# Transposes one step later, later ranking stages, an earlier x split, and cluster rows moved and partly made on ScalarE, in a fused attention and two-MLP kernel

## The chip, the cores and the metric

The kernel runs on one core of one Trainium2 chip. The metric is the device time of one execution in microseconds; three runs of the kernel before gave 794.3, 794.31 and 795.95. TensorE is called PE in the profile, VectorE DVE, ScalarE ACT, GpSimd POOL and SyncE SP.

## The reference, cut to what matters

Attention runs on 2 batches of 8 heads with 768 tokens and head size 64. Each query and key is given to the cluster (of 16) whose normalised centroid it is nearest to; a query sees only keys of its own cluster. The 1536 tokens then pass two MLPs in fp32.

```python
q_assign = argmax(q_n @ c_n)          # k_assign likewise, per head
scores = where(q_assign == k_assign, scale * q @ k.T, -1e9)
attn = softmax(scores) @ v
h = x @ w_in                          # x: attention output, 1536 x 512; w_in 512 x 2048
g = P(h) / Q(h)                       # P cubic, Q = 1 + |b0||h| + |b1|h^2
x2 = g @ w_out                        # 2048 x 512
out = (silu(x2 @ w_gate) * (x2 @ w_val)) @ w_out2
```

## The kernel before, in words

Every fp32 operand is split into a high part that the matmul takes exactly and a low part (the rest), and products are summed from two or three matmuls.

**Steps.** The attention phase is one loop over steps, from -18 to 107, written out on all five engines. Step i makes the scores of tile i: head i // 6, 128 queries by 768 keys (96 tiles in all). The other stages of a tile follow some steps later. Within one step TensorE goes through: scores of tile i (L1226, L1229), the six transposes of tile i - LAG (L1239), the PV matmuls of a group (L1254, L1256), the transposes of is_top (L1278), the rank matmul (L1292), one half of a head's centroid logits (L1313), and from step 96 to 103 half a unit of the first MLP's hidden product (L1109 to L1111, asked for by TAIL_CHUNKS). A group is three tiles; its PV runs in three steps, beginning at PV_LAG = LAG + 3 behind its first tile.

**VectorE in a step:** at some steps the cluster rows (L1024, L1026), the row maximum neg_max (L1035), every third step the sums row_den and reciprocals row_inv of three tiles (L1046, L1049), the low parts probT_lo of the transposed tile (L1057, two halves), at the end of a group x_raw (L1066), and the stages of the next head: logit sum and top (L1072, L1074), is_top (L1080). **ScalarE in a step:** exp of tile i - 1 (L811), the copy topT (L819), the high parts probT_hi (L829, two halves), x_part at the end of a group (L839), logit_lo (L861). **POOL:** normalisation of three tiles (L589), the splits of q and k (L597 to L606), of v (L614, L617), of MLP weights (L624, L626), and of a finished pair of heads x (L636, L638).

**What ties them.** The transposes of a tile write the two PT banks of PSUM, so they wait until probT_lo of the tile before has read each half (s_pT_lo), and for the normalisation (s_norm). The first PV matmul of a group waits for the low parts of its last tile and for x_raw of the group before (s_xsum). The maximum waits for the scores, exp for the maximum, and the scores of tile i for exp of tile i - 2.

**Head stages.** `head_at(step, stage)` says which head is in a stage: step = 6 h - 18 + stage + late. Stages are the split (0), logits (6 and 7), their sum (8), is_top (9), its transpose (10), the rank matmul (11) and the cluster rows (12). The rank matmul gives, for each query and key, -0.5 in the row of its first best centroid and 0 or more elsewhere. The cluster rows are made of it: 1 or 0 for q, -2^96 or 0 for k. SP sends them in six transfers per head to qk_low (L390), where they are part of the score matmul's operands. The logits and the rank product lie in one PSUM bank, so the logits of the next head wait for the cluster rows (s_cluster).

**The end of attention.** TAIL puts the activation of hidden units 0 and 1 into steps 98 and 100, on ScalarE (hidden_read, L685 to L693), VectorE (mlps, L925 to L953) and POOL (mlp1, L516); TAIL_LOG puts their logarithm and the high part g_hi (hidden_finish, L711 to L726) into steps 99 and 101. The first result matmul, first_result(0), follows the loop and waits for the last x_raw, since its results take the attention's PSUM banks. In a step, each engine does the attention's work ahead of this.

Of the kernel before, what the change touches and what calls it, by code (L numbers as in the profile page):

```python
# [21 lines left out]
def build_program(nc, q, k, v, centroids, w_in, w_out1, a, b, w_gate, w_val, w_out2, out):  # L22
    P = 128
# [5 lines left out]
    T = S // P  # L29
# [185 lines left out]
    def sem(name):  # L215
        return nc.alloc_semaphore(name)
# [22 lines left out]
        "s_pT", "s_pT_hi", "s_pT_lo", "s_pv", "s_xhi", "s_xlo"))  # L239
    s_w1p_hi, s_w1p, s_w1hi, s_w1lo = (sem(x) for x in ("s_w1p_hi", "s_w1p", "s_w1hi", "s_w1lo"))  # L240
# [16 lines left out]
    LAG = 5  # L257
    PV_LAG = LAG + HALF
    V_STEP = 3
    X_STEP, LAST_X_STEP = 5, 2  # L260
# [7 lines left out]
    def head_at(step, stage):  # L268


        for h in range(NH):
            late = -4 * (h == 1) + (h == 2 and stage <= S_SUM)
            if T * h + late == step + PREP_LEAD - stage:
                return h
        return None

    def tile_at(step):
        return step if 0 <= step < NT else None
# [85 lines left out]
    with block:  # L364

        @block.sync
        def _(sp):
# [19 lines left out]
            def send_cluster(h):  # L387
                sp.wait_ge(s_cluster, 2 * h)
                for t in range(T):
                    sp.dma_start(*cluster_rows(h, t)).then_inc(s_clrows[h % 3], 16)  # L390
# [88 lines left out]
        def _(pool):  # L479
# [103 lines left out]
            for step in STEPS:  # L583
# [45 lines left out]
                if pv_at(step - LAST_X_STEP) == (NG - 1, HALF - 1):  # L629
                    g1, third = NG - 1, HALF - 1  # L630
# [27 lines left out]
        def _(sc):  # L658
# [144 lines left out]
            for step in STEPS:  # L803

                i = tile_at(step - 1)
# [68 lines left out]
        def _(ve):  # L874
# [136 lines left out]
            for step in STEPS:  # L1011
# [8 lines left out]
                elif h is not None:  # L1020
                    ve.wait_ge(s_rank, h + 1)
                    if h > 1:
                        ve.wait_ge(*clustered(h - 1))
                    v_.tensor_scalar(clusterT[0:T * C, 0, :], rank_out[0:T * C, 0:P], 0.0, 1.0,  # L1024
                                     ALU.is_lt, ALU.mult).then_inc(s_cluster, 1)
                    v_.tensor_scalar(clusterT[0:T * C, 1, :], rank_out[0:T * C, P:2 * P], 0.0, -BIG,  # L1026
                                     ALU.is_ge, ALU.mult).then_inc(s_cluster, 1)
                i = tile_at(step)
                if i is not None:

                    ve.wait_ge(s_score, i + 1)
                    if i >= T:
# [3 lines left out]
                                     ALU.max, negate=True).then_inc(s_max, 1)  # L1036
                if (step - HALF) % HALF == 0 and 0 <= (step - HALF) // HALF < NG:
# [61 lines left out]
        def _(pe):  # L1099
# [110 lines left out]
            for step in STEPS:  # L1210
# [85 lines left out]
                for n in range(2):  # L1296
# [9 lines left out]
                    if h == 0:  # L1306
                        pe.wait_ge(s_cen, 1)
                    elif h > 1:
                        pe.wait_ge(s_cluster, 2 * (h - 1))
# [67 lines left out]
```

## Time and profile before

| | |
|---|---|
| median of three runs | 794.31 us |
| the profiled execution | 794.28 us |
| its span, first to last instruction | 792.5 us |
| TensorE busy | 781.2 us (99%) |
| VectorE busy | 571.9 us (72%) |
| ScalarE busy | 517.3 us (65%) |
| POOL busy | 522.7 us (66%) |
| granted TensorE clock, mean | 0.996 of full |

A row of a timeline gives the start in us from the span's start, the duration, the engine, the line, the operation, and the tile written and those read with their shapes; x6 means six instructions merged into one row. In brackets stands the idle time of the engine before the row and what ended it. Matmuls overlap in the pipeline and their ends are modelled, so their start times are what can be trusted. PEld is the load of weights, SPq the time in which SP issues a transfer.

### The profile page before, as it was taken

The numbers are of one execution on the slowest core, as the hardware profiler recorded it, in microseconds if no ns is written. First come the engines' busy times: TensorE is split into PE (matmuls) and PEld (weight loads), VectorE is DVE, ScalarE is ACT, GpSimd is POOL, SyncE is SP. The second block draws the span as 40 slices with busy tenths as digits, with TensorE's granted clock in tenths as the row PEclk, the third lists the DMA queues.
The fourth block names the chain that finished last, engine by engine and source line by source line (L and its number), as shares of the span: only waits on it lengthen the run. The fifth ranks groups of instructions, "written<-read, shape, count | busy, mean of one in ns | idle before, by whom it ended". The sixth has DMA issues, their size and how long they took to land.

```text
span 792.5 us, 12617 instructions
## 1 busy us (share of the span) xinstructions
PE 781.2 (99%) x4204; PEld 697.7 (88%) x4204; DVE 571.9 (72%) x1043; ACT 517.3 (65%) x957; POOL 522.7 (66%) x457
## 2 busy tenths in 40 slices
PE   8999999999999999999999999999999999999998
PEld 7799999999998888888888888899999999999997
DVE  5899999999997888778777777745445545554453
ACT  4888888888887787777767889744444444333322
POOL 4767988998575799322222288888889876655620
PEclk8999999999999999999999999999999999999999
DMA  8776555454310700000000011241111114111102
GB/s 206 180 199 162 143 140 125 116 145 121 85 60 19 221 28 0 1 1 1 1 1 0 1 55 54 66 147 50 32 54 53 37 45 134 54 28 53 28 1 80
DMA packets 57681, 57.92 MB, mean 73 GB/s; under 512 B 6608, under 2 KB 44304, under 8 KB 57616
## 3 DMA queue, kind: packets, MB, share of 16 engines
q1 hardware_dynamic: 57376, 56.52, 26.6%
q8 instruction: 34, 0.56, 0.3%
q10 hardware_dynamic: 240, 0.59, 0.3%
q14 instruction: 31, 0.25, 0.1%
HBM read 33.59 MB, written 3.15 MB: 46 GB/s over the span
## 4 chain that ended last, share of the span: by engine, by line
PE 87%; DVE 8%; issue 2%; ACT 2%; DMA 0%; DVEq 0%; ACTq 0%
PE ps L1111 18%; PE ps L1109 18%; PE ps L1110 18%; PE ps L1239 6%; PE ps L1204 4%; PE ps L1205 4%; PE ps L1203 4%; DVE neg_max L1035 3%; DVE probT_lo L1057 3%; PE ps L1254 3%; PE ps L1226 3%; PE ps L1256 3%; PE ps L1313 2%; PE ps L1229 2%; ACT prob L811 1%
## 5 line engine op out<-in xcount | busy, mean ns | idle before, releaser
L516 POOL TENSOR_TENSOR den<-den,mag 128x512 f32<-128x512 f32 x48 | 62.3, 1298 | 121.8 <-ACT den L689 121.6
L1111 PE MATMUL ps<-x_hi,w_lo 128*128 128x512 f32 (+1 forms) x384 | 139.5, 363 | 0.0
L1109 PE MATMUL ps<-x_hi,w_hi 128*128 128x512 f32 (+1 forms) x384 | 139.4, 363 | 0.0
L1110 PE MATMUL ps<-x_lo,w_hi 128*128 128x512 f32 (+1 forms) x384 | 139.3, 363 | 0.0
L575 POOL TENSOR_TENSOR w_lo<-w_raw,w_hi 128x768 fp32r<-128x768 f32 (+1 forms) x48 | 101.6, 2125 | 56.4 <-ACT w_hi L742 56.4
L589 POOL TENSOR_SCALAR prob<-prob,row_inv 128x768 f32<-128x768 f32 x96 | 85.6, 907 | 39.2 <-DVE row_inv L1049 38.7
L829 ACT ACTIVATE probT_hi<-ps 128x384 fp32r<-128x384 f32 x192 | 84.2, 489 | 25.9 <-PE ps L1239 24.2
L1057 DVE TENSOR_TENSOR probT_lo<-ps,probT_hi 128x384 fp32r<-128x384 f32 x192 | 96.8, 545 | 5.3 <-ACT probT_hi L829 4.0
L1035 DVE TENSOR_REDUCE neg_max<-ps 128x1 f32<-128x768 f32 x96 | 91.1, 950 | 8.8 <-PE ps L1229 8.5
L811 ACT ACTIVATE prob<-ps,neg_max 128x768 f32<-128x768 f32 x96 | 86.8, 905 | 10.8 <-DVE neg_max L1035 10.1
L1239 PE MATMUL ps<-ident,prob 128*128 128x128 f32 x576 | 81.7, 277 | 4.4 <-DVE probT_lo L1057 4.1
L1239 PEld LDWEIGHTS ps<-ident,prob 128*128 128x128 f32 x576 | 65.6, 140 | 17.0 <-issue 9.9
L1109 PEld LDWEIGHTS ps<-x_hi,w_hi 128*128 128x128 f32 x384 | 72.1, 188 | 8.2
L1110 PEld LDWEIGHTS ps<-x_lo,w_hi 128*128 128x128 f32 x384 | 72.1, 188 | 8.2
L1111 PEld LDWEIGHTS ps<-x_hi,w_lo 128*128 128x128 f32 x384 | 72.1, 188 | 7.5
L1111 PE MATMUL ps<-g_hi,w_lo 128*128 128x512 f32 x192 | 74.8, 390 | 0.0
L1110 PE MATMUL ps<-g_lo,w_hi 128*128 128x512 f32 x192 | 74.8, 390 | 0.0
L1109 PE MATMUL ps<-g_hi,w_hi 128*128 128x512 f32 x192 | 74.8, 390 | 0.0
L1254 PE MATMUL ps<-probT_hi,v_split 128*128 128x384 f32 x192 | 72.5, 378 | 0.0
L763 ACT ACTIVATE act_hi<-ps 128x384 fp32r<-128x384 f32 x48 | 23.6, 492 | 64.6 <-DVE ps L992 43.7
L1256 PE MATMUL ps<-probT_lo,v_split 128*128 128x384 f32 x192 | 64.6, 337 | 0.0
L959 DVE TENSOR_TENSOR sum<-ps,gate 128x384 f32<-128x384 f32 x24 | 13.4, 557 | 68.9 <-PE ps L1111 68.9
(145 smaller groups left out, 1987.5 us busy)
## 6 DMA issues: line engine op xcount, KB each, us to landing
k_hihi<-qk_hi SPq DMA_DIRECT2D x32, 192.0 KB, 4.0
w_raw<-in_moe_w_gate SPq DMA_DIRECT2D x48, 128.0 KB, 2.3
w_raw<-in_moe_w_val SPq DMA_DIRECT2D x48, 128.0 KB, 2.5
w_raw<-in_moe_w_in SPq DMA_DIRECT2D x16, 256.0 KB, 3.7
w_raw<-in_moe_w_out SPq DMA_DIRECT2D x16, 256.0 KB, 5.0
qk_raw<-in_q SPq DMA_DIRECT2D x16, 192.0 KB, 3.4
q_hilo<-qk_hi SPq DMA_DIRECT2D x16, 192.0 KB, 3.4
qk_low<-qk_hi SPq DMA_DIRECT2D x16, 192.0 KB, 4.5
```

The source lines that it names most:

```text
L575: did(g.tensor_tensor(lo[:, wave, :], raw[:, wave, :], hi[:, wave, :].bitcast(F32), ALU.subtract), s_w2lo)
L589: did(g.tensor_scalar(prob[i][:, :], prob[i][:, :], row_inv[:, i:i + 1], 1.0, ALU.mult, ALU.mult), s_norm)
L811: s.activation(prob[i % T][:, :].rearrange("p (c n) -> p c n", c=2), ps[:, bank:bank + 2, 0:HC], ACT.Exp, bias=neg_max[:, i % T:i % T + 1] ...
L829: s.activation(probT_hi[g % 2][:, n * HALF:(n + 1) * HALF, c:c + P], ps[:, PT_BANK + n, 0:HC].rearrange("p (k n) -> p k n", k=HALF), ACT.C ...
L1035: v_.tensor_reduce(neg_max[:, i % T:i % T + 1], ps[:, bank:bank + 2, 0:HC], AX.XY, ALU.max, negate=True).then_inc(s_max, 1)
L1057: v_.tensor_tensor(probT_lo[g % 2][:, keys, c:c + P], ps[:, PT_BANK + n, 0:HC].rearrange("p (k n) -> p k n", k=HALF), probT_hi[g % 2][:, k ...
L1109: mm(dst, hi, m_hi, start=start, stop=False)
L1110: mm(dst, hi, m_lo, start=False, stop=False)
L1111: return mm(dst, lo, m_hi, start=False, stop=stop)
L1239: last = transpose(ps[:, PT_BANK + n, kt % HALF * P:(kt % HALF + 1) * P], prob[i % T][:, kt * P:(kt + 1) * P], ident[:, :])
L1254: mm(ps[:, O_BANK, 0:HC], vv, probT_hi[g % 2][:, kt, :], start=(kt == 0), stop=False)
L1256: last = mm(ps[:, O_BANK, 0:HC], vv, probT_lo[g % 2][:, kt, :], start=False, stop=(kt == T - 1))
```

## The change

LAG goes from 5 to 6: the transposes, the high and low parts and PV of each tile come one step later, and the loop has one step more. For heads 2 and later, the stages from the logits on come one step later than 6 h - 18 + stage (for head 2 that was so up to the logit sum), and the split keeps its step. The x pairs are split one step after their last PV, where it was five (two for the last pair). The q cluster rows are made by ScalarE as Relu(-2 x), ahead of exp, with a new semaphore s_qrow; the k rows stay on VectorE, but behind the maximum of the step, and wait for s_qrow. s_cluster now counts one per head. Nothing else in the loop is changed; TAIL, TAIL_LOG and TAIL_CHUNKS keep their steps.

```diff
--- before.py
+++ after.py
@@ -237,6 +237,7 @@
         "s_score", "s_max", "s_exp", "s_den", "s_inv", "s_norm"))
     s_pT, s_pT_hi, s_pT_lo, s_pv, s_xhi, s_xlo = (sem(x) for x in (
         "s_pT", "s_pT_hi", "s_pT_lo", "s_pv", "s_xhi", "s_xlo"))
+    s_qrow = sem("s_qrow")
     s_w1p_hi, s_w1p, s_w1hi, s_w1lo = (sem(x) for x in ("s_w1p_hi", "s_w1p", "s_w1hi", "s_w1lo"))
     s_w2sum, s_w2hi, s_w2lo, s_wohi, s_wolo = (sem(x) for x in (
         "s_w2sum", "s_w2hi", "s_w2lo", "s_wohi", "s_wolo"))
@@ -254,10 +255,10 @@
 
     R_LAG = 3
     COPIES, CLROWS = 16 * 6, 16 * T
-    LAG = 5
+    LAG = 6
     PV_LAG = LAG + HALF
     V_STEP = 3
-    X_STEP, LAST_X_STEP = 5, 2
+    X_STEP = 1
     PREP_LEAD = 18
     FIRST_STEP = -PREP_LEAD
     S_SPLIT, S_CEN, S_LOGIT, S_SUM, S_TOP, S_TOPT, S_RANK, S_CLUSTER = 0, 2, 6, 8, 9, 10, 11, 12
@@ -269,7 +270,9 @@
 
 
         for h in range(NH):
-            late = -4 * (h == 1) + (h == 2 and stage <= S_SUM)
+            late = -4 * (h == 1)
+            if h >= 2:
+                late = 1 if stage >= S_LOGIT else int(h == 2)
             if T * h + late == step + PREP_LEAD - stage:
                 return h
         return None
@@ -385,7 +388,7 @@
                     sp.dma_start(dst, src).then_inc(s_copy[h % 3], 16)
 
             def send_cluster(h):
-                sp.wait_ge(s_cluster, 2 * h)
+                sp.wait_ge(s_cluster, h)
                 for t in range(T):
                     sp.dma_start(*cluster_rows(h, t)).then_inc(s_clrows[h % 3], 16)
 
@@ -626,8 +629,6 @@
                     did(g.tensor_tensor(w1_lo[u][:, :], w1_raw[u][:, :], w1_hi[u][:, :].bitcast(F32),
                                     ALU.subtract), s_w1p)
                 g1, third = pv_at(step - X_STEP)
-                if pv_at(step - LAST_X_STEP) == (NG - 1, HALF - 1):
-                    g1, third = NG - 1, HALF - 1
                 if third == HALF - 1 and g1 % 4 == 3:
                     pool.wait_ge(s_xsum, g1 + 1)
                     finish_last()
@@ -802,6 +803,13 @@
 
             for step in STEPS:
 
+                h = head_at(step, S_CLUSTER)
+                if h:
+                    sc.wait_ge(s_rank, h + 1)
+                    if h > 1:
+                        sc.wait_ge(*clustered(h - 1))
+                    s.activation(clusterT[0:T * C, 0, :], rank_out[0:T * C, 0:P], ACT.Relu, scale=-2.0
+                                 ).then_inc(s_qrow, 1)
                 i = tile_at(step - 1)
                 if i is not None:
                     sc.wait_ge(s_max, i + 1)
@@ -1017,14 +1025,6 @@
                         v_.tensor_scalar(qk_low[0][0:C, g, :].rearrange("c (t n) -> c t n", t=T)[:, cols, :],
                                          rank_rows[:, cols, g, :], 0.0, worth, op, ALU.mult
                                          ).then_inc(s_row0, 1)
-                elif h is not None:
-                    ve.wait_ge(s_rank, h + 1)
-                    if h > 1:
-                        ve.wait_ge(*clustered(h - 1))
-                    v_.tensor_scalar(clusterT[0:T * C, 0, :], rank_out[0:T * C, 0:P], 0.0, 1.0,
-                                     ALU.is_lt, ALU.mult).then_inc(s_cluster, 1)
-                    v_.tensor_scalar(clusterT[0:T * C, 1, :], rank_out[0:T * C, P:2 * P], 0.0, -BIG,
-                                     ALU.is_ge, ALU.mult).then_inc(s_cluster, 1)
                 i = tile_at(step)
                 if i is not None:
 
@@ -1034,6 +1034,11 @@
                     bank = score_bank(i)
                     v_.tensor_reduce(neg_max[:, i % T:i % T + 1], ps[:, bank:bank + 2, 0:HC], AX.XY,
                                      ALU.max, negate=True).then_inc(s_max, 1)
+                h = head_at(step, S_CLUSTER)
+                if h:
+                    ve.wait_ge(s_qrow, h)
+                    v_.tensor_scalar(clusterT[0:T * C, 1, :], rank_out[0:T * C, P:2 * P], 0.0, -BIG,
+                                     ALU.is_ge, ALU.mult).then_inc(s_cluster, 1)
                 if (step - HALF) % HALF == 0 and 0 <= (step - HALF) // HALF < NG:
 
                     half = (step - HALF) // HALF
@@ -1306,7 +1311,7 @@
                     if h == 0:
                         pe.wait_ge(s_cen, 1)
                     elif h > 1:
-                        pe.wait_ge(s_cluster, 2 * (h - 1))
+                        pe.wait_ge(s_cluster, h - 1)
                     centers = cenT[:, h % H, :, :].rearrange("p n c -> p (n c)")
                     for t in range(n * HALF, (n + 1) * HALF):
                         for x in (qk_hi, qk_lo):
```

## Rows read from the trace of the kernel before

**Rows 1.** TensorE's timeline over a head in mid-attention: start us, us, engine line op out<-in

```profile
101.83 0.82 PE L1239 MATMUL ps<-ident,prob 128*128 128x128 f32 x6
...
104.57 0.82 PE L1239 MATMUL ps<-ident,prob 128*128 128x128 f32 x6
...
106.63 0.82 PE L1239 MATMUL ps<-ident,prob 128*128 128x128 f32 x6
...
109.05 0.92 PE L1239 MATMUL ps<-ident,prob 128*128 128x128 f32 x6 [0.21 <-DVE probT_lo L1057]
...
113.75 0.91 PE L1239 MATMUL ps<-ident,prob 128*128 128x128 f32 x6
...
115.03 0.19 PEld L1313 LDWEIGHTS ps<-cenT,qk_hi 128*128 128x128 f32 x1
```

**Rows 2.** VectorE's timeline, of a head before and of the same head

```profile
97.20 0.94 DVE L1035 TENSOR_REDUCE neg_max<-ps 128x1 f32<-128x768 f32 x1
98.29 1.02 DVE L1057 TENSOR_TENSOR probT_lo<-ps,probT_hi 128x384 fp32r<-128x384 f32 x2
...
112.05 0.96 DVE L1035 TENSOR_REDUCE neg_max<-ps 128x1 f32<-128x768 f32 x1
113.04 1.02 DVE L1057 TENSOR_TENSOR probT_lo<-ps,probT_hi 128x384 fp32r<-128x384 f32 x2
113.98 0.28 DVE L1024 TENSOR_SCALAR clusterT<-ps 96x128 fp32r<-96x128 f32 x1
...
114.37 0.94 DVE L1035 TENSOR_REDUCE neg_max<-ps 128x1 f32<-128x768 f32 x1
115.24 0.15 DVE L1046 TENSOR_REDUCE row_den<-row_sum 128x3 f32<-128x6 f32 x1
...
115.51 0.99 DVE L1057 TENSOR_TENSOR probT_lo<-ps,probT_hi 128x384 fp32r<-128x384 f32 x2
```

**Rows 3.** ScalarE's timeline in the same head

```profile
112.10 0.37 ACT L819 ACTIVATE topT<-ps 96x256 fp32r<-96x256 f32 x1
112.37 0.86 ACT L829 ACTIVATE probT_hi<-ps 128x384 fp32r<-128x384 f32 x2
```

**Rows 4.** SyncE's queue in the same head: one issue line for six transfers

```profile
103.27 3.88 SPq L390 DMA_DIRECT2D qk_low<-clusterT  x6
```

**Rows 5.** VectorE's and TensorE's timelines at the start of attention

```profile
22.70 0.94 DVE L1035 TENSOR_REDUCE neg_max<-ps 128x1 f32<-128x768 f32 x1
...
28.71 0.92 PE L1239 MATMUL ps<-ident,prob 128*128 128x128 f32 x6
```

**Rows 6.** timelines of TensorE, ScalarE and VectorE at the end of attention, steps 95 to 99

```profile
240.92 0.82 PE L1239 MATMUL ps<-ident,prob 128*128 128x128 f32 x6
...
243.05 0.92 PE L1239 MATMUL ps<-ident,prob 128*128 128x128 f32 x6 [0.47 <-DVE probT_lo L1057]
...
248.64 0.82 PE L1239 MATMUL ps<-ident,prob 128*128 128x128 f32 x6
...
249.92 0.61 ACT L685 ACTIVATE mag<-ps 128x512 f32<-128x512 f32 x1
...
253.46 1.01 DVE L1057 TENSOR_TENSOR probT_lo<-ps,probT_hi 128x384 fp32r<-128x384 f32 x2
```

**Rows 7.** timelines of VectorE and TensorE from step 100 to the first result

```profile
256.92 0.69 DVE L925 SCALAR_TENSOR_TENSOR den<-den,ps 128x512 f32<-128x512 f32 x1
...
260.42 0.68 DVE L953 TENSOR_TENSOR g_lo<-ps,g_hi 128x512 fp32r<-128x512 f32 x1
...
261.29 0.33 PE L1254 MATMUL ps<-probT_hi,v_split 128*128 128x384 f32 x1
...
262.70 0.56 DVE L1066 TENSOR_TENSOR x_raw<-ps,x_part 64x384 f32<-64x384 f32 x1 [1.59 <-ACT x_part L839]
...
263.41 0.47 PE L1109 MATMUL ps<-g_hi,w_hi 128*128 128x512 f32 x1
```

**Rows 8.** groups of instructions by line, ScalarE: count, busy us, mean ns, idle before

```profile
L663 ACT ACT_TABLE_LOAD x1 | 1.3, 1283 | 1.4 <-PEq L1358 1.4
```

## The prediction

> **What bounds the kernel now.** I read the page first. It shows TensorE busy nearly all the time, but matmul ends are modelled, so that number hides waits of some tenths of a us; only start times show them. So I took the timelines of TensorE, VectorE and ScalarE over one head of attention, then the start and the end of attention. From the first result matmuls of the hidden layer on, nothing is touched by the change, and those 529 us stay.
>
> In attention each step starts its six transposes at a time that I call T. A plain step costs TensorE 2.06 us (104.57 to 106.63), one with half of a head's logits 2.74 (101.83 to 104.57) [rows 1]. The two steps from 104.57 to 109.05 take 4.48 where TensorE has 4.12 of work: the row at 109.05 says that the transposes wait for VectorE, whose low halves (probT_lo) free their PSUM bank. A head takes 14.7 us, of which I count 14.0 as TensorE's work (six plain steps 12.4, logits 1.4, an estimated 0.3 for the transposes and the product of the ranking). So 0.7 per head, at most 9 us in 13 regular heads, could be won. VectorE sets the time in the four steps with the logit sum, is_top and both x_raw; TensorE sets it in the two with the logits (T = 113.75 and the next). A saving helps only in the first kind, a late signal hurts in both.
>
> **The change, as places.** LAG 6 and the later head stages both shift by one step, so transposes, PV, logits, top and rank keep their order against one another: a step of after looks like the step before it in the old kernel. What moves against this pattern is the scores and maxima (one tile ahead), the row sums with their reciprocals, and the cluster rows. I number the places by the old step modulo 6: T = 113.75 is place 0, T = 109.05 place 4.
>
> **Row sums** (two small VectorE instructions, 0.27 us, 115.24 to 115.51 [rows 2]) leave places 0 and 3 for 5 and 2. From 3 to 2 they stay on the same VectorE stretch, the 4.48: nothing. From 0, where TensorE sets the time, to 5, where VectorE does: a cost. At place 5 the low half starts 0.99 behind the maximum (112.05 to 113.04) in one parity of heads and 1.09 (97.20 to 98.29) in the other; maximum and row sums together take 0.87 (114.37 to 115.24) and 0.27, that is 1.14 [rows 2]. So 0.15 and 0.05, mean 0.10. In 13 heads 1.3 us. In the last two heads, where VectorE sets every step, the sums use up small waits for ScalarE: I estimate -0.3.
>
> **Cluster rows.** Both leave VectorE's place 0 (0.39, 113.98 to 114.37 [rows 2]). They are covered there by the logits, so taking them away gives nothing. ScalarE's Relu reads 96x128. No row shows it; nearest is ScalarE's 96x256 copy, which holds the engine 0.27 (112.10 to 112.37 [rows 3]). I take 0.27, ends 0.2 (VectorE's price) and 0.45. It stands behind the rank matmul and ahead of an exponential, which comes up to 0.4 later; the scores that need it come 2 us behind it: nothing on the path. If that cover is gone, 0.4 per head.
> The k rows now come behind the maximum, and the next head's logits wait for them (s_cluster). With the low half started at 113.04, VectorE is free at 113.98, has the maximum at 114.85, the k rows (0.28) at 115.13 and the signal at about 115.23 [rows 2]. TensorE loads the first logit weights at 115.03 [rows 1], 0.20 too early. Part of that is hidden, since weights are loaded ahead of the matmul that uses them, while the last PV matmul still runs: I take 0.13 per head, ends 0 and 0.3. In 13 heads: 1.7 us.
>
> The Trainium skill, "ScalarE: Activation LUTs", section "Rules for kernel authors", says to do relu on VectorE and not on ScalarE. By that rule the q rows would be dearer after the change, as the rows put it too (0.27 against 0.2); the sum is the same by either, since neither price lies on the path.
>
> **x pairs.** POOL makes them three steps earlier, off the step in which they delay the next normalisation, and the transposes come one step later behind that. POOL isn't what TensorE waits for now, so nothing won; nothing lost either, since each group of three steps on POOL becomes shorter or stays. If they still delayed a normalisation, it has a step of 2.3 more.
> **SP.** The six cluster transfers go out from 103.27 on, 3.9 us, although their rows were ready near 99.7: copies are ahead of them [rows 4]. The scores that read them come near 113, 5.9 later than the last issue; the change takes one step of 2.3 of that. Nothing; if the rest is used up by landing, up to 1 us per head.
>
> **Start.** Step 3 loses is_top to step 4, so maximum 4 starts at 22.30 and not at 22.70 [rows 5]. Then by the prices above: maximum 0.95, exponential 1.02, signal 0.08, scores 0.90: maximum 6 at 25.25; with row sums (1.14) to 26.39; low half 0.94 to 27.33; maximum 0.87, k rows 0.28, signal 0.12: logits at 28.60; logits and scores 1.37: T of tile 2 at 29.97. Before: 28.71 [rows 5]. Cost 1.3, bounds 0 and 2.
>
> **End,** the largest term. The diff leaves TAIL, TAIL_LOG and TAIL_CHUNKS where they are, while transposes and PV end one step later.
> (1) T of step 96 in after has place 95 of before, 240.92. From step 96 to 98: 5.59 as before (243.05 to 248.64) [rows 6].
> (2) In step 98 ScalarE now has x_part ahead of the first hidden read. x_raw, behind x_part, starts 1.41 after its PV group (261.29 to 262.70 [rows 7]), PV 0.57 to 0.65 after T. So the read starts at T+2.06, where it was T+1.28 (248.64 to 249.92). From the read to the low half of the step after 3.54 (249.92 to 253.46) [rows 6], 0.54 for its first part, 0.13 signal: T of step 100 comes 6.27 behind that of step 98, 0.75 more than TensorE needs.
> (3) In step 100 VectorE does the activation of n=1, 4.2 us (256.92 to 260.42 plus 0.68) [rows 7]. Before, no low half was left behind it. Now tile 95's is, and then x_raw, and the last group's first PV waits for both: low half of tile 94 done at T+2.07, activation to 6.27, low half 1.0, x_raw 0.56, signal 0.15: T+7.98. TensorE is there at T+5.53: a wait of 2.45.
> (4) Two PV groups with their hidden chunks, 2.1 each, then the last PV group, behind which no chunk is left. Before, a chunk covered the way x_part, x_raw, first result (261.29 to 263.41, 2.12) [rows 7]; now 1.43 of that is open.
> Sum: 5.59 + 6.27 + 7.98 + 2.1 + 2.1 + 2.12 = 26.15; before 263.41 - 240.92 = 22.49. The open waits are 4.6, and 1.0 goes that before had around step 96 (the row at 243.05 shows 0.47 of it [rows 6]). Cost 3.7; bounds 1.4 (only (4)) and 5.
>
> **Sum:** 1.3 + 1.3 - 0.3 + 1.7 + 3.7 = 7.7 us. The profiled execution took 794.28 (span 792.5 and 1.8 around it), the median of the runs is 794.31, so no correction. Forecast 802.0.
>
> **Rivals.**
> A. The steps of attention come out even: late k rows and row sums fall into slack that I misread by 0.2 us. Start and (4) alone give 794.3 + 1.3 + 1.4 = 797.0, with the whole end 799.3. For it: both costs are near the length of a signal. Chance 0.20.
> B. Faster. The wait at 109.05 is not for the low halves but for POOL's normalisation, or VectorE's full queue as a whole, and the extra step with 0.2 us less VectorE per head dissolves it: 0.37 x 14 = 5.2 won, against 2.7 for start and (4): 791.8. It is decided at place 4: T must come sooner than 4.48 behind the T two steps before, by over 0.2 per head to pay for the end. Against: the tile transposed there was normalised several steps earlier, and the row names the low half. Chance 0.11.
> C. Relu brings table loads. One is 1283 ns [rows 8]; two per head are 2.6 on a ScalarE that has some 12.4 of 14.7 busy. That is at least 0.6 over, and 2.6 where it meets place 5: in 15 heads 811 to 841. Against: Copy and Abs share Exp's table now, with three loads in all. Chance 0.04. The Trainium skill, "ScalarE: Activation LUTs", section "Table sets: the hidden batching unit", says that relu is in every set; no run here shows it.
> D. A queue slips: SP's cluster transfers, or the exponential behind Relu, meet the scores, 0.3 to 0.5 per head more: 806 to 808. Chance 0.10.
> The forecast (both attention terms and the end as worked out) has 0.55.
>
> **How the numbers follow.** 0.2% (1.6 us) is about what a measurement of this kernel can tell from no change. The forecast's own range: attention 0 to 5, start and end 3 to 7, so 798 to 805. With A and half of D 796 to 806, which leaves out B, C and the rest of D. Slower: the forecast, C, D and most of A, 0.83. Same: what is left of A and B, 0.07. Faster: 0.10.
>
> **What would show it.** Six steps of T 14.9 to 15.0 and not 14.7; the first logit weight load about 0.2 us behind its place, waiting for clusterT; at place 5 row_den between maximum and low half. Relu near 0.3 us on ScalarE and three table loads as now. At the end: about 2.4 us of wait ahead of the PV group of step 102, VectorE's last low half behind g_lo, and some 1.4 ahead of the first result matmul, which starts near 271. It would be wrong if a head takes 14.7 or less, or if the wait at step 102 is absent.

## The result and the profile after

The kernel after takes 805.61 us (median of five runs, 804.09 to 807.79) against 794.31 for the kernel before (five runs, 794.23 to 795.96): a ratio of 1.013 with a 95% interval of 1.0107 to 1.0154. That is slower, and inside the range of 796 to 806, though 3.6 us above the number forecast and just above the 798 to 805 that the forecast gave as its own range. The profiled execution took 806.47, with a span of 804.7 against 792.5.

The page of the kernel after: its span, and the busy time of each engine.

```profile
span 804.7 us, 12617 instructions
...
PE 788.6 (98%) x4204; PEld 697.6 (87%) x4204; DVE 568.8 (71%) x1028; ACT 519.0 (64%) x972; POOL 523.4 (65%) x457
```

TensorE is again busy for nearly the whole span. VectorE's work is 3 us less and ScalarE's 2 us more (Relu has moved there), and yet the span is 12.2 longer: busy shares explain nothing here, and start times have to. I therefore compared T, the start of a tile's transposes, for all 96 tiles in both traces. From the first result matmul on nothing differs: it starts at 275.52 and not at 263.41 [rows 7], 12.1 later, which is the whole loss.

The steps of attention, after: TensorE's timeline over the same head as [rows 1].

```profile
101.14 0.82 PE L1244 MATMUL ps<-ident,prob 128*128 128x128 f32 x6
...
103.33 0.90 PE L1244 MATMUL ps<-ident,prob 128*128 128x128 f32 x6
...
104.80 0.19 PEld L1318 LDWEIGHTS ps<-cenT,qk_hi 128*128 128x128 f32 x1 [0.20 <-issue]
...
106.28 0.82 PE L1244 MATMUL ps<-ident,prob 128*128 128x128 f32 x6
...
109.01 0.82 PE L1244 MATMUL ps<-ident,prob 128*128 128x128 f32 x6
...
111.06 0.90 PE L1244 MATMUL ps<-ident,prob 128*128 128x128 f32 x6
...
113.50 0.92 PE L1244 MATMUL ps<-ident,prob 128*128 128x128 f32 x6
```

The step with the first logits takes 106.28 - 103.33 = 2.95, where the same step of the same head took 2.82 before (all such steps before: 2.79 to 2.83; after: 2.95 to 2.98). The row of the weight load shows why: it comes 0.20 late. The next three steps (2.73, 2.05, 2.44) are as before. In particular T at place 4 still comes 4.49 behind the T two steps before it, where it was 4.48.

VectorE's timeline, after: the maximum with the k rows behind it, and the row sums at place 5 of the next head.

```profile
103.54 0.95 DVE L1035 TENSOR_REDUCE neg_max<-ps 128x1 f32<-128x768 f32 x1
104.41 0.28 DVE L1040 TENSOR_SCALAR clusterT<-ps 96x128 fp32r<-96x128 f32 x1
...
116.49 0.96 DVE L1035 TENSOR_REDUCE neg_max<-ps 128x1 f32<-128x768 f32 x1
117.48 0.16 DVE L1051 TENSOR_REDUCE row_den<-row_sum 128x3 f32<-128x6 f32 x1
...
117.77 0.53 DVE L1062 TENSOR_TENSOR probT_lo<-ps,probT_hi 128x384 fp32r<-128x384 f32 x1
```

At place 5 the low half now starts 1.28 behind the maximum, where it was 0.99 [rows 2].

All instructions on the cluster rows, after: count, duration in ns (min, median, max), first and last start.

```profile
L811 ACT ACTIVATE clusterT<-ps x15: 273/275/282, 15.4 to 222.9; 96x128 fp32r<-96x128 f32 x15
L1040 DVE TENSOR_SCALAR clusterT<-ps x15: 269/277/279, 15.7 to 224.4; 96x128 fp32r<-96x128 f32 x15
```

Two single steps lose more than all regular logits together. The first is between tiles 5 and 6: TensorE, SP's queue and the late weights, after.

```profile
33.53 4.14 SPq L393 DMA_DIRECT2D qk_low<-clusterT  x6
...
36.59 0.92 PE L1244 MATMUL ps<-ident,prob 128*128 128x128 f32 x6
...
39.00 0.30 PEld L1231 LDWEIGHTS ps<-k_hihi,q_hilo 128*128 128x128 f32 x2 [0.83 <-issue]
...
39.82 0.82 PE L1244 MATMUL ps<-ident,prob 128*128 128x128 f32 x6
```

The second is between tiles 19 and 20: TensorE and VectorE in step 25, after (VectorE's first rows are the end of its step 24).

```profile
71.78 0.55 DVE L1062 TENSOR_TENSOR probT_lo<-ps,probT_hi 128x384 fp32r<-128x384 f32 x1
72.03 0.90 PE L1244 MATMUL ps<-ident,prob 128*128 128x128 f32 x6
72.25 0.48 DVE L1090 TENSOR_SCALAR par<-par 128x4 f32<-128x4 f32 x1
...
72.82 0.78 DVE L1093 TENSOR_TENSOR par<-par 128x2 f32<-128x2 f32 x1
...
73.53 0.95 DVE L1035 TENSOR_REDUCE neg_max<-ps 128x1 f32<-128x768 f32 x1
...
74.40 0.27 DVE L1040 TENSOR_SCALAR clusterT<-ps 96x128 fp32r<-96x128 f32 x1
...
74.82 0.27 PE L1318 MATMUL ps<-cenT,qk_hi 128*128 128x64 f32 x1 [1.18 <-DVE clusterT L1040]
...
76.27 0.82 PE L1244 MATMUL ps<-ident,prob 128*128 128x128 f32 x6
```

Three small instructions that prepare the MLP's parameters, once in the whole kernel, run from 72.25 to 73.5. They stand ahead of the maximum and so of the k rows, and the step takes 4.24 where it took 2.80. Two of the three are mostly held up: the first (128x4) takes 0.48 and the last (128x2) 0.78, where the middle one takes 0.15. Both end within 0.03 us of the end of an instruction of POOL (72.71 and 73.59, in the normalisation), and so does every one of them that takes over 0.2 in any of the 13 profiles. So what they cost depends on what POOL is doing beside them; experiments 6 and 9 show it.

The end, after: timelines of TensorE and VectorE from step 100 to the first result.

```profile
259.68 0.52 PE L1244 MATMUL ps<-ident,prob 128*128 128x128 f32 x3 [0.65 <-DVE probT_lo L1062]
...
265.23 0.69 DVE L961 TENSOR_TENSOR g_lo<-ps,g_hi 128x512 fp32r<-128x512 f32 x1
265.84 1.01 DVE L1062 TENSOR_TENSOR probT_lo<-ps,probT_hi 128x384 fp32r<-128x384 f32 x2
266.88 0.56 DVE L1071 TENSOR_TENSOR x_raw<-ps,x_part 64x384 f32<-64x384 f32 x1
267.59 0.41 PE L1259 MATMUL ps<-probT_hi,v_split 128*128 128x384 f32 x1 [2.15 <-DVE x_raw L1071]
...
271.15 0.50 PE L1259 MATMUL ps<-probT_hi,v_split 128*128 128x384 f32 x1
...
275.52 0.47 PE L1114 MATMUL ps<-g_hi,w_hi 128*128 128x512 f32 x1 [1.26 <-DVE x_raw L1071]
```

Here stand the three waits of the prediction: 0.65 at step 100, 2.15 ahead of the PV group of step 102, 1.26 ahead of the first result. The 3.56 from 267.59 to 271.15 are new. That is one PV group and its hidden chunk, 2.1 in the kernel before. Stretches of 3 us, after: busy time of PE, PEld, DVE, ACT and POOL, then the granted clock, DMA share and GB/s.

```profile
265.00:268.00 3.00, 0.85 (x4) 0.45 (x4) 2.41 (x5) 1.41 (x3) 2.31 (x1) 1.00 0.93 267
268.00:271.00 3.00, 3.00 (x10) 2.54 (x9) 0.00 (x0) 0.00 (x0) 0.00 (x0) 0.51 0.69 229
271.00:274.00 3.00, 3.00 (x15) 2.58 (x14) 0.00 (x0) 0.00 (x0) 0.00 (x0) 0.92 0.00 0
```

Behind the wait the granted clock is 0.51 for some 3 us, the lower of its two levels (1.2 GHz of 2.4), and costs 3.56 - 2.1 = 1.46. That belongs to this execution: in three other profiles with the same wait the clock stays at 1.00 (experiment 8).

**Where 12.1 us went,** as changes of T between the two traces. The measured parts add up to the shift; the forecast's to 7.5, since it counted 13 heads with a first logit half where these stretches have 12:

| stretch | predicted | measured |
|---|---|---|
| start, to T of tile 2 | 1.3 | 1.36 |
| tiles 2 to 5 | 0 | -0.10 |
| tiles 5 to 6 | 0 | 0.83 |
| place 0, the regular 11 heads | 1.4 | 1.65 |
| place 0, tile 19 to 20 | 0.1 | 1.44 |
| other places, tiles 6 to 79 | 1.3 | 1.29 |
| last two heads, tiles 79 to 90 | -0.3 | 0.05 |
| T of tile 90 to the first result | 3.7 | 5.59 |

### The profile page after: what moved, and what is told of

It reads as the page before. It is cut to its first block, busy times and chain, and to the rows that moved or that the text cites. A ratio compares the mean times of both kernels' runs of the same rounds, so it can differ in the third digit from the quotient of the medians.

```text
span 804.7 us, 12617 instructions
## 1 busy us (share of the span) xinstructions
PE 788.6 (98%) x4204; PEld 697.6 (87%) x4204; DVE 568.8 (71%) x1028; ACT 519.0 (64%) x972; POOL 523.4 (65%) x457
## 3 DMA queue, kind: packets, MB, share of 16 engines
q1 hardware_dynamic: 57376, 56.52, 26.2%
## 4 chain that ended last, share of the span: by engine, by line
PE 88%; DVE 7%; issue 3%; ACT 1%; DMA 0%; DVEq 0%
PE ps L1114 18%; PE ps L1116 18%; PE ps L1115 18%; PE ps L1244 6%; PE ps L1209 4%; PE ps L1210 4%; PE ps L1208 4%; PE ps L1231 3%; DVE probT_lo L1062 3%; PE ps L1259 3%; PE ps L1234 3%; PE ps L1318 3%; PE ps L1261 3%; DVE neg_max L1035 2%; PE ps L1283 0%
```

## The experiments

**1. The cluster rows back on VectorE** ahead of the maximum, with their waits and counts as they were, in the kernel after. The theory: 0.13 per head and the 1.3 of step 25 are the price of the k rows behind the maximum. The rival: Relu or the shifted stages cost it.

```diff
-                    s.activation(clusterT[0:T * C, 0, :], rank_out[0:T * C, 0:P], ACT.Relu, scale=-2.0
-                                 ).then_inc(s_qrow, 1)
...
+                    v_.tensor_scalar(clusterT[0:T * C, 0, :], ..., ALU.is_lt, ALU.mult).then_inc(s_cluster, 1)
+                    v_.tensor_scalar(clusterT[0:T * C, 1, :], ..., ALU.is_ge, ALU.mult).then_inc(s_cluster, 1)
                 i = tile_at(step)
```

> The changed kernel with both cluster rows again on VectorE ahead of the maximum, nothing else touched. Theory (terms add up at their places): the logits no longer wait for the k rows, so 0.15 us per head goes in 13 heads, and the 1.3 us that the logits of step 25 wait behind the parameter instructions of step 24 stays only if the rows stay behind them: rows ahead of the maximum are still behind those instructions, but the maximum (0.87) is out of the way, so some 0.9 of 1.4 goes. About 0.4 at the start. Together 3.2 us: 802.4. Rival 1 (ScalarE's Relu is what costs, by delaying the exponentials): the same gain, but the wait would leave ScalarE's exp and not the first logit weight load. Rival 2 (one step more of lag costs in every head, whatever the rows do): within 1 us of 805.6.

Measured: 803.4 (ratio 1.0108, 1.0092 to 1.0124), span 802.1. The direction is right and the size 2.2 to 2.6 instead of 3.2. The regular step with the first logits is back at 2.82. The step of tile 19 only falls from 4.24 to 3.57: the parameter instructions still delay the rows, since these are made in the step behind them. The start shows 0.36 less at T of tile 2, although tile 0 came 0.31 later in this profile: between tiles 0 and 2 it is 0.67 less.

**2. The same rows alone in the kernel before:** Relu on ScalarE, k rows behind the maximum, nothing else.

```diff
+                    s.activation(clusterT[0:T * C, 0, :], rank_out[0:T * C, 0:P], ACT.Relu, scale=-2.0
+                                 ).then_inc(s_qrow, 1)
...
                                      ALU.max, negate=True).then_inc(s_max, 1)
+                    ve.wait_ge(s_qrow, h)
+                    v_.tensor_scalar(clusterT[0:T * C, 1, :], ..., ALU.is_ge, ALU.mult).then_inc(s_cluster, 1)
```

> The kernel before with only the cluster rows as in the change: q rows by ScalarE's Relu, k rows behind the maximum. Theory: at place 0 the logits wait for the k rows, 0.15 us per head in 13 heads, 2 us in all. In step 24 the parameter instructions come behind the k rows of the same step here (place 0 is step 24, not 25), so the 1.4 us of the changed kernel do not show. 796.3. Rival (Relu, or the rank wait at the head of ScalarE's queue, costs besides): 798 or more. Rival (the cost needs the longer lag): 794.4.

Measured: 798.29 (1.0044, 1.0029 to 1.0059), span 796.6. Place 0, TensorE and VectorE of the kernel before with the new rows:

```profile
103.10 0.28 DVE L1040 TENSOR_SCALAR clusterT<-ps 96x128 fp32r<-96x128 f32 x1
103.49 0.19 PEld L1318 LDWEIGHTS ps<-cenT,qk_hi 128*128 128x128 f32 x1 [0.19 <-issue]
```

The wait is the same 0.2, the step goes from 2.80 to 2.95 in every head, and 1.7 us comes of that between tiles 6 and 79. All other places there are as before within 0.05, but for one step that is 0.15 shorter. This isolates the term: k rows behind the maximum cost 0.14 per head. At the start they cost more: from T of tile 0 to T of tile 2 it takes 4.92 and not 4.21. Another 2.0 of the 4.0 us in this profile were there already when T of tile 0 came (26.49 against 24.50); its granted clock was 0.79 in the stretch from 20 to 26, against 1.00 in the profile of before, and the first scores came 0.4 later. I take those 2.0 for the scatter of the start and not for an effect of the rows; no run separates the two.

**3. The end's tables shifted by one step,** in the kernel after.

```diff
-    TAIL_CHUNKS = {NT + n: ((2 * n) // DC, (2 * n) % DC) for n in range(AHEAD * DC // 2)}
-    TAIL = {NT + 2: 0, NT + 4: 1}
-    TAIL_LOG = {NT + 3: 0, NT + 5: 1}
+    TAIL_CHUNKS = {NT + 1 + n: ((2 * n) // DC, (2 * n) % DC) for n in range(AHEAD * DC // 2)}
+    TAIL = {NT + 3: 0, NT + 5: 1}
+    TAIL_LOG = {NT + 4: 0, NT + 6: 1}
```

> The changed kernel with TAIL, TAIL_LOG and TAIL_CHUNKS one step later, as the transposes and PV are. Theory: the end of attention is then what it was in place, the waits of 0.8, 2.3 and 1.4 us and the half clock behind the second of them (1.5 us) go, and the wait of about 1 us in step 96 comes back: 5.6 us less, 800.0, with the first result matmul 22.5 us behind the transposes of tile 90. Rival (the loop's extra step is itself the cost, or x_raw of the last group): under 2 us less, 804.

Measured: 800.44 (1.0077, 1.0058 to 1.0096), span 798.7: 5.2 less than after. The first result follows its chunk with no wait, and the clock stays at 1.00. From T of tile 90 to the first result it takes 22.79, where it took 22.49 before the change and 28.08 after it. TensorE's timeline, the last matmul of the chunk and the first result:

```profile
269.30 0.40 PE L1116 MATMUL ps<-x_hi,w_lo 128*128 128x512 f32 x1
269.56 0.47 PE L1114 MATMUL ps<-g_hi,w_hi 128*128 128x512 f32 x1
```

So the end's cost comes from three tables of steps that were not moved with LAG.

**4. The row sums one step later,** in the kernel after, so that they leave place 5 again. The same edit is made for POOL's normalisation.

```diff
-                if (step - HALF) % HALF == 0 and 0 <= (step - HALF) // HALF < NG:
-                    half = (step - HALF) // HALF
+                if (step - HALF - 1) % HALF == 0 and 0 <= (step - HALF - 1) // HALF < NG:
+                    half = (step - HALF - 1) // HALF
```

> The changed kernel with row sums, reciprocals and the normalisation one step later, so back at their old place beside the transposes. Theory: place 5 loses 0.24 us in every second head, which is 1.2 to 1.5 us less: 804.3. Nothing more, since at place 3 they stand on the same VectorE stretch as at place 2. Rival (POOL's normalisation now limits the transposes of place 4, where the profile names it 13 times): it comes 2.3 us later for the same tile, so the wait there grows, 806 or more.

Measured: 808.62 (1.0179, 1.0155 to 1.0204), span 806.9: slower, not faster. A miss that is instructive. In the middle the edit does what it should: from tile 12 to tile 90 it takes 2.0 less than after, place 5 is back at its old lengths (2.33, and 2.17 to 2.22 in the other parity), and in the last two heads the steps of 2.60 are 2.30 again. But at the start it adds 4.8 in the steps from tile 2 to 5. TensorE and POOL of this kernel there:

```profile
32.89 0.83 POOL L600 TENSOR_SCALAR qk_raw<-qk_raw 64x768 f32<-64x768 f32 x1 [4.81 <-DMA qk_raw<-in_k]
...
34.72 1.80 POOL L609 TENSOR_TENSOR qk_lo<-qk_raw,qk_hi 128x768 fp32r<-128x768 f32 x1
36.50 1.79 POOL L592 TENSOR_SCALAR prob<-prob,row_inv 128x768 f32<-128x768 f32 x2
...
37.46 0.76 PE L1244 MATMUL ps<-ident,prob 128*128 128x128 f32 x5 [3.35 <-POOL prob L592]
```

POOL's normalisation of tiles 3 to 5 came, one step later, behind the split of the next head in POOL's queue. That split waits 4.81 for its transfer, and everything behind it waits with it. The step with the wait is 3.5 longer; the two behind it are 1.3 longer in sum, in part at a granted clock of 0.5, from 38.5 to 41.9. The number is in the rival's range (806 or more), but not for the rival's reason: place 4 stays at 2.37 to 2.40.

**5. All three undone:** the edits of 1, 3 and 4 together.

> The three edits together: of the change only LAG 6 and the later head stages are left, and the earlier x split. Theory: place by place this is the old kernel, so a head takes 14.74 us again, and what stays over it is the start (1.0 to 1.3 us) and the wait of the second head's scores for its cluster transfers (0.8): 796.2. Rival (lag costs per head): 798 or more.

Measured: 801.87 (1.0089, 1.0073 to 1.0105), span 800.7, the same miss: tiles 2 to 5 take 12.1, where they take 6.6 before and 6.5 after the change. Behind it, from tile 22 on, the shift against before stays between 7.8 and 8.25 up to tile 95: with rows, sums and tail undone, LAG 6 itself costs nothing in the regular steps.

**6. The same, with the sums one step later only from group 6 on,** when POOL's transfers no longer bind.

```diff
+                due = (step - HALF) if step < HALF * (GLATE + 1) else (step - HALF - 1)
+                if due % HALF == 0 and 0 <= due // HALF < NG and (due // HALF < GLATE or step > HALF * (GLATE + 1)):
+                    half = due // HALF
```

> The changed kernel with TAIL and its partners one step later, both cluster rows ahead of the maximum, and the row sums one step later from the seventh group of three tiles on (the first six at the step they have in the change, ahead of POOL's splits). Theory: the 5.7 us by which the run with all sums later missed was POOL's queue at the start, where the sums' normalisation came behind a split that waits for its transfer; without it remain the start 1.0 to 1.4, the transfers of head 2 0.8 and 0.9 in step 25 behind the parameter instructions: 797.4. In the middle a head takes 14.74 us as before. Rival (the miss was something else of the longer lag): 799 or more, or a middle that differs.

Measured: 797.66 (1.0038, 1.0024 to 1.0052), span 797.7. Tiles 2 to 5 take 6.5 again. The profiled execution took 799.50, 1.8 above the median. The change with three parts undone is still above the kernel before: 0.8 between tiles 5 and 6, 0.2 between tiles 6 and 19, 1.6 between tiles 19 and 20, nothing more behind that up to the first result, and a start that was 2.6 later at tile 0 in this profile. The 1.6 were forecast as 0.9. VectorE's third parameter instruction and POOL, in this run:

```profile
73.41 1.82 POOL L611 TENSOR_TENSOR qk_lo<-qk_raw,qk_hi 128x768 fp32r<-128x768 f32 x1
73.45 1.80 DVE L1092 TENSOR_TENSOR par<-par 128x2 f32<-128x2 f32 x1
```

The same instruction takes 0.78 in after, and 0.16 in experiments 4 and 5, where POOL's subtraction has ended by then. Here it ends with that subtraction, 1.80 later, and the cluster rows stand behind it.

The late start is one at the lower clock, though the profile gives 1.00: its record of the clock begins at 17.6, where the others begin near 5. TensorE's first logits in this run:

```profile
7.43 0.40 PE L1317 MATMUL ps<-cenT,qk_lo 128*128 128x64 f32 x1
7.64 0.40 PE L1317 MATMUL ps<-cenT,qk_hi 128*128 128x64 f32 x1
```

They start 0.21 apart, and 0.11 apart in after at the same place (7.01 and 7.12), where its clock is 1.00.

**7. The parameters one step later,** in the kernel after.

```diff
-                if step == 4 * T:
+                if step == 4 * T + 1:
```

> The changed kernel with the three parameter instructions of VectorE (about 1.3 us) in step 25 behind the low halves, and no longer in step 24, where they stand between the low halves and the maximum whose k rows the logits wait for. Theory: the wait of 1.48 us of step 25 falls to the 0.2 of the other heads, and VectorE has the room at the next place: 1.2 to 1.3 us less, 804.3. Rival (that wait is for SP's transfers or the rank matmul): no change in it.

Measured: 804.7 (1.0123, 1.01 to 1.0145), span 801.6. Tiles 19 to 20 take 2.97, as a regular head, and not 4.24: the 1.27 is shown in the trace. The medians differ by 0.9, less than the spread of either kernel's runs. TensorE's timeline ahead of the PV group of step 102:

```profile
266.05 0.41 PE L1259 MATMUL ps<-probT_hi,v_split 128*128 128x384 f32 x1 [2.14 <-DVE x_raw L1071]
```

Its clock is 1.00 behind that wait, though the wait is as long as in the kernel after.

**8. The wait filled:** nine 128x512 matmuls on loaded data, their result not used, ahead of the PV group of step 102.

```diff
+                    if g == NG - 1 and third == 0:
+                        for _ in range(9):
+                            mm(ps[:, PREP, :], w1_hi[0][:, 0:P], x_hi[:, 0, 0:TB], start=True, stop=True)
```

> The changed kernel with nine matmuls of 512 columns, whose result nothing reads, put ahead of the first PV matmul of the last group (2.1 us, in a wait of 2.3). They change neither that wait's end nor any operand. Theory: the granted clock does not fall behind the wait, so the PV group and the hidden chunk there take 2.1 us and not 3.56: 1.4 us less, 804.2, with the first result matmul 1.4 sooner. Rival (the slow stretch comes from something else than the idle time): no change or 0.2 more.

Measured: 805.66 (1.0135, 1.0115 to 1.0156), span 802.6. The stretch in which after stood at 0.51:

```profile
268.00:271.00 3.00, 3.00 (x16) 2.56 (x15) 0.00 (x0) 0.00 (x0) 0.00 (x0) 1.00 0.38 131
```

The clock holds and the group with its chunk takes 2.16. From T of tile 90 to the first result it takes 26.55. But the clock also held in the profiles of experiments 4, 7 and 10, which filled nothing (26.50 to 26.53 for the same stretch), and the median did not fall. Of six profiles with the wait unfilled, three show the lower clock (after, 1 and 9) and three don't. So the profile of this run can't show that the filling kept the clock up: inconclusive.

**9. The x pairs back at their old step,** in the kernel after.

```diff
-                g1, third = pv_at(step - X_STEP)
+                g1, third = pv_at(step - (X_STEP if step > NT else 4))
```

> The changed kernel with the x pairs three steps later again, at the step number they had (the last pair stays). Theory: POOL is not what TensorE waits for, so every interval between transposes stays within 0.05 us and the time within the spread, 805.6. Rival (the earlier x pairs gave something back, which hid a larger loss): the normalisation behind them comes 1.5 us later and the transposes three steps on wait, 0.3 to 1 us in each of seven pairs, 808 or more.

Measured: 806.59 (1.0139, 1.0121 to 1.0157), span 804.7, as after. T of tile 95 comes at 262.50, against 262.53. The steps stay within 0.05 but for two. Tiles 5 to 6 take 2.77 and not 3.23, which scatters (experiment 10). Tiles 19 to 20 take 3.97, and 4.22 to 4.28 in after and in experiments 3, 4, 8 and 10, which leave the x pairs, the rows and the parameters as they are. There the earlier x pair ends on POOL at 71.69 in after and puts the normalisation back, and VectorE's first parameter instruction, which ends with the normalisation's first, takes 0.48 and not the 0.21 of this run. So the earlier x pairs cost 0.27 in that one step and nothing elsewhere.

**10. SP's two parameter loads** taken from ahead of the loop to behind the cluster transfers of head 2.

```diff
-            sp.dma_start(a_raw, a[None, :].to_broadcast([P, 4])).then_inc(s_par_in, 16)
-            sp.dma_start(b_raw, b[None, :].to_broadcast([P, 2])).then_inc(s_par_in, 16)
...
+                if h == 3:
+                    sp.dma_start(a_raw, a[None, :].to_broadcast([P, 4])).then_inc(s_par_in, 16)
+                    sp.dma_start(b_raw, b[None, :].to_broadcast([P, 2])).then_inc(s_par_in, 16)
```

> The changed kernel with the two parameter loads (1.1 us of SP's queue) behind the cluster transfers of head 2 and not ahead of them. Theory: the scores of tile 12 wait for these transfers, since they come one step sooner against them than before; the interval from the transposes of tile 5 to those of tile 6 falls from 3.23 to about 2.4 us, and the time by 0.8: 804.8. Rival (they wait for POOL's split of that head or the exponential): interval unchanged.

Measured: 806.34 (1.0136, 1.0119 to 1.0154), span 804.8. Tiles 5 to 6 take 2.39, as before the change, and not 3.23. I don't put that down to the edit: in this profile attention began 2.5 later (T of tile 0 at 27.58 against 25.08) and the last issue ended only 0.7 later (38.41 against 37.67), which gave the transfers 1.8 more cover. And the kernels of experiments 3 and 8, whose SP queue is untouched, show 2.49 and 2.37 in their profiles. In experiment 3 the transfers were issued 0.7 earlier. SP's queue and the weights of the scores in experiment 3:

```profile
32.79 4.17 SPq L393 DMA_DIRECT2D qk_low<-clusterT  x6
...
38.30 0.30 PEld L1231 LDWEIGHTS ps<-k_hihi,q_hilo 128*128 128x128 f32 x2
```

From the end of the last issue (36.96) to the weights are 1.34, without a wait; in after it is 39.00 - 37.67 = 1.33, with one; in experiments 1, 6 and 9 it is 1.32 to 1.34, with one, and in experiment 7 2.45, with one of 0.53. So the transfers' landing fits as what binds, though no edit shows it, and how much of it binds differs between executions, from nothing to 0.8. What sets its length stays open.

**11. A version faster than both.** In the kernel before, VectorE sets the time at place 3, and the sum over two columns (the accumulated row sum and the column beside it with 1e-9) is a separate instruction. This leaves that addition out: the reciprocal reads the row sums themselves.

```diff
-                    v_.tensor_reduce(row_den[:, c:c + HALF], row_sum[:, c:c + HALF, :], AX.X, ALU.add
-                                     ).then_inc(s_den, 1)
-                    ve.wait_ge(s_den, half + 1)
-                    v_.reciprocal(row_inv[:, c:c + HALF], row_den[:, c:c + HALF]).then_inc(s_inv, 1)
+                    v_.reciprocal(row_inv[:, c:c + HALF], row_sum[:, c:c + HALF, 0]).then_inc(s_inv, 1)
```

> The kernel before with the reciprocal taken straight from the sums that exp accumulates: the addition of 1e-9 is left out, which fp32 rounds away beside a sum that holds exp(0) = 1. One VectorE instruction of 0.18 us less per group of three tiles. Theory (VectorE sets the time at place 3 and in the last two heads): 0.18 in 13 heads and in the 5 last groups, 3.2 us less, 791.1; at place 0 nothing. Rival (POOL's normalisation is what the transposes of place 4 wait for): under 1 us less, since POOL's own time stays.

Measured: 791.64 against 795.22 for the kernel before on the same chip (0.9955, 0.9937 to 0.9972), span 790.1. VectorE's and TensorE's timelines around place 3 of this kernel:

```profile
105.51 0.82 PE L1236 MATMUL ps<-ident,prob 128*128 128x128 f32 x6
106.11 0.95 DVE L1035 TENSOR_REDUCE neg_max<-ps 128x1 f32<-128x768 f32 x1
106.98 0.17 DVE L1046 RECIPROCAL row_inv<-row_sum 128x3 f32<-128x3 f32 x1
107.06 0.99 DVE L1054 TENSOR_TENSOR probT_lo<-ps,probT_hi 128x384 fp32r<-128x384 f32 x2
107.74 0.92 PE L1236 MATMUL ps<-ident,prob 128*128 128x128 f32 x6
```

The low half starts 0.95 behind the maximum instead of 1.14, and the step takes 2.23 instead of 2.42 [rows 1]: the 0.19 arrives in full, 2.5 us between tiles 6 and 79. One step at the start, tile 6 to 7, gives 0.6 back; why is not settled. At place 0, where the same instruction goes too, twelve steps together gain 0.12. The last two heads give 0.2 and not the 0.9 of the theory. The first result is 2.87 earlier; 0.73 of that is there at tile 6, 0.32 of it already at tile 0, where the start scatters. It confirms the picture from the other side: a saving on VectorE is worth its length at place 3 and nothing at place 0.

## Why the prediction was right, and where it fell short

**Right.** The kernel is slower, by the mechanisms forecast and at their places, which give some 8 of the 12.1 us in the profiles.
- *Start:* T of tile 2 was forecast at 29.97 and came at 30.07, and the steps on the way came as worked out (maximum 6 at 25.28 for 25.25, first logits at 28.63 for 28.60). That the profiles before and after both began early is luck: T of tile 0 scatters by more than the term.
- *K rows:* forecast 0.13 per head, from a load that stood 0.20 ahead of the rows' signal; measured 0.14 to 0.15 from a load 0.20 late, alone in experiment 2 and undone in experiment 1.
- *End:* the open waits were forecast as 0.75, 2.45 and 1.43 and are 0.65, 2.15 and 1.26. The time from T of step 100 to the PV group of step 102 is 7.91 against 7.98. Experiment 3 takes all three away.
- *Relu* takes 275 ns, as taken from ScalarE's copy, and the profile after has the same three table loads as before. Rival C is out. The trace agrees here with the Trainium skill, "ScalarE: Activation LUTs", section "Table sets: the hidden batching unit", which has relu in every table set. The Trainium skill's section "Rules for kernel authors" on the same page gives relu to VectorE and not to ScalarE, with a figure for bf16; for this fp32 tile from PSUM, relu on ScalarE was no dearer than the compare-and-multiply on VectorE (275 against 277 ns for the same shape).
- *Rival B* is out: place 4 still comes 4.49 behind the T two steps before. *Rival A* is out: the nine heads from tile 20 to tile 74 take 15.02 each, where they took 14.75.

**Right in sum, not in its parts: the row sums.** Forecast 0.15 and 0.05 in alternate heads; measured 0.24 and 0.01 at place 5. The step "maximum and row sums together take 0.87 and 0.27" took the 0.87 from a place where the next instruction follows at once. At place 5 in this parity of heads the instruction behind a maximum starts 0.99 after it, as [rows 2] already show; 0.99 + 0.27 = 1.26, and 1.28 was measured. In the other parity the old gap of 1.09 was a wait for ScalarE that took in the sums. Places 2 and 3 are 0.09 more and 0.09 less in alternate heads, and one step there is 0.14 less, the one in which the parameter instructions stood before. The total is 1.29, against 1.3: that it fits so well is luck.

**Wrong: four steps that together gave 4.4 us too little.**
- *"In 13 heads: 1.7 us"* took every head to be like the one read. In step 25 the k rows stand behind the parameter instructions of step 24 as well, 1.3 more; experiment 7 takes it away. Of this 0.27 is the x pairs' (experiment 9), which the prediction had at nothing. I moved the k rows and looked at what was queued ahead of them in one head, not in each.
- *"SP ... Nothing; if the rest is used up by landing, up to 1 us per head"* holds for the head read, with 5.9 between the last issue and the scores. For head 2, the first that goes by the new shift, the scores come 1.33 behind the last issue. Rival D had the mechanism, but as a cost per head and not of one head: 0.83 here, from nothing to 0.8 over the profiles.
- *The end as 3.7.* Of the 5.59, 1.46 is the group at half clock, which I had not in the sum; 0.35 is in the steps 96 to 98, which I took to be as before; 0.15 in the second group. In the three profiles with this wait whose clock held (4, 7 and 10) the end costs 4.0.
- *"In the last two heads ... I estimate -0.3"*: it is 0.05. The two steps that take the row sums in (tiles 84 and 87) went from 2.31 and 2.35 to 2.60 and 2.61; the gains in others only balance them. Experiment 4 gives 0.5 back.

Of these the 1.3 (but for its share of the x pairs) and the room for the 0.8 were readable in the trace before. The fall of the clock was not: the kernel before has no wait that long in attention.

**Open.** What decides whether the clock falls behind the wait. Half of the profiles with it show the fall, and the kernels' medians don't separate by it. For a link speaks that the clock falls nowhere else: between the start and the end of the kernel the 13 profiles have six falls, each from 0.8 before to 1.2 us behind the end of a wait of TensorE: three of 2.14 or 2.15 us (after, 1 and 9), one each of 3.35 and 2.80 (experiments 4 and 5) and one of 1.14 (experiment 2, at 23.5). Waits of 1.2 us in other profiles had none. The start scatters too: T of tile 0 lies between 24.2 and 27.6 in the profiles, with the first scores between 15.2 and 17.9. That goes with the clock at the start. In the eight profiles with T of tile 0 up to 25.7 the clock is at 1.00 from 16.6 at the latest; in four with 26.2 and later it stays near 0.5 until 17.6 to 18.2 (in experiment 6 by the pace of the matmuls), and in experiment 2 it falls a second time. Why it stays low longer in some executions is open. That scatter is as large as several terms of the sum, so I have read single terms from intervals of T and not from medians.

## What to carry to other kernels

When a stage of a software pipeline moves by one step, look for the tables that count steps on their own (here three constants of the tail, 3.7 to 5.3 us by the profiles) and for the queues in which something stands once (parameters, a first head, a first transfer): the regular steps were forecast to 0.1 us, and nearly all that was missed lay in single steps. Behind an in-order engine a moved instruction costs what now stands ahead of it in its worst step, and a later one may fall behind a wait for a transfer, as POOL's normalisation did in experiment 4. Read the place from start times before saving: 0.19 us of VectorE were worth 0.19 per head at place 3 and nothing at place 0.

## What was not expected of the hardware

The granted clock fell to 0.51 for some 3 us behind 2.15 us without matmuls, in three of six executions with that wait; it had been at 1.00 since 17 us at the latest. VectorE's arithmetic on 128x4 and 128x2 elements takes 0.15 to 0.16 us alone and up to 1.80 beside POOL, and then ends within 0.03 us of a POOL instruction. A weight load that comes 0.20 late costs the step 0.14 to 0.15; before the change that load ran beside the last PV matmul, which started at the same 115.02. An instruction behind the same 128x768 maximum starts 0.86 to 0.88 after it, or 0.99 in two of twelve steps, and the profile doesn't say why.
